# Attention with a shared score tile for the last queries of two heads, and a new order of all engines

## The reference, cut to what matters

```python
batch, n_heads, seq, head_dim = (4, 8, 576, 64)          # float32
scores = scale * np.matmul(q, k.transpose(0, 1, 3, 2))
cum = np.cumsum(np.maximum(s, 0.0), axis=-1)
bias = -(cum[:, :, :, None] - cum[:, :, None, :])
scores = np.where(causal, -1000000000.0, scores + np.minimum(bias, 0.0))
attn = np.exp(scores - np.max(scores, axis=-1, keepdims=True))
attn = attn / (np.sum(attn, axis=-1, keepdims=True) + 1e-09)
return np.matmul(attn, v).astype(np.float32)
```

## Time and profile before

| | us |
|---|---|
| median of 3 runs (lowest, highest) | 879.79 (879.1, 881.36) |
| the profiled execution | 881.97 |
| its span, first to last instruction | 880.2 |
| TensorE busy | 775.4 |
| VectorE busy | 486.0 |
| ScalarE busy | 378.7 |
| GpSimd busy | 163.6 |

### The profile page before, as it was taken

The page is one execution under the profiler, slowest core; times in us unless marked ns, Lnnn a source line. Parts: engine busy times, 40 slices in busy tenths (PEclk is TensorE's granted clock), DMA queues, the critical chain, the costliest instruction groups (busy, mean ns, idle before and its releaser), DMA issues.

```text
span 880.2 us, 15547 instructions
## 1 busy us (share of the span) xinstructions
PE 775.4 (88%) x4885; PEld 649.7 (74%) x4886; DVE 486.0 (55%) x947; ACT 378.7 (43%) x846; POOL 163.6 (19%) x341
## 2 busy tenths in 40 slices
PE   2778888788888999999999997579999999999993
PEld 2566667566676899989899895458888888887772
DVE  8577777877775363453462353854644663726221
ACT  2576676766765340431431512334442551533110
POOL 4134454532222100000000000021122122221121
PEclk9999999999999999999999998579999999999997
DMA  6622232222210000010010012961543561611110
GB/s 156 192 57 57 58 71 54 54 64 57 64 26 23 3 1 1 1 54 0 0 54 0 0 55 71 365 239 38 222 164 119 206 235 49 225 32 34 41 42 16
DMA packets 81405, 70.41 MB, mean 80 GB/s; under 512 B 61960, under 2 KB 61960, under 8 KB 81322
## 3 DMA queue, kind: packets, MB, share of 16 engines
q1 hardware_dynamic: 77354, 58.49, 21.6%
q0 software_dynamic: 4000, 11.28, 3.9%
HBM read 59.72 MB, written 11.86 MB: 81 GB/s over the span
## 4 chain that ended last, share of the span: by engine, by line
PE 82%; DVE 10%; ACT 3%; issue 2%; DMA 1%; SPq 0%; POOL 0%; POOLq 0%; ACTq 0%; DVEq 0%
PE sbank L1091 25%; PE sbank L1684 10%; PE sbank L1686 9%; PE sbank L1685 9%; PE obank L837 5%; PE tbank L806 5%; PE sbank L786 4%; DVE nmax L661 3%; PE sbank L788 3%; PE obank L1139 2%; ACT probs L551 1%; DVE q L653 1%; PE tbank L1669 1%; PE tbank L1709 1%; PE sbank L793 1%
## 5 line engine op out<-in xcount | busy, mean ns | idle before, releaser
L551 ACT ACTIVATE probs<-sbank,nmax 128x128 f32<-128x128 f32 (+4 forms) x160 | 90.6, 568 | 62.3 <-DVE nmax L661 60.8
L806 PE MATMUL tbank<-ident,probs 128*128 128x128 f32 x480 | 75.7, 279 | 20.5 <-ACT pT L558 20.1
L786 PE MATMUL sbank<-k,q 128*128 128x256 f32 (+2 forms) x192 | 74.4, 393 | 16.3 <-ACT probs L551 14.7
L661 DVE TENSOR_REDUCE nmax<-sbank 128x1 f32<-128x128 f32 (+4 forms) x160 | 80.1, 532 | 7.5 <-PE sbank L793 5.9
L1684 PE MATMUL sbank<-w_high,xsT_h 128*128 x184 | 75.0, 407 | 1.9 <-DVE xsT_l L1609 1.7
L1193 DVE TENSOR_TENSOR w_low<-w_low,w_high (+1 forms) x64 | 74.0, 1218 | 0.7 <-ACT w_high L1549 0.3
L1686 PE MATMUL sbank<-w_low,xsT_h 128*128 x184 | 72.7, 395 | 0.0
L1685 PE MATMUL sbank<-w_high,xsT_l 128*128 x184 | 72.5, 394 | 0.0
L1684 PE MATMUL sbank<-w_high,hidT_h 128*128 x176 | 71.0, 403 | 0.1
L806 PEld LDWEIGHTS tbank<-ident,probs 128*128 128x128 f32 x480 | 51.1, 141 | 25.7 <-ACT pT L558 23.9
L1549 ACT CAST w_high<-w_low (+1 forms) x64 | 62.3, 1053 | 17.5 <-SPq L1438 17.5
(11 more groups left out here) (246 smaller groups left out, 1939.7 us busy)
## 6 DMA issues: line engine op xcount, KB each, us to landing
w_low<-in_moe_w_dram SPq DMA_DIRECT2D x16, 2048.0 KB, 14.1
k_raw<-in_k_dram SPq DMA_DIRECT2D x32, 128.0 KB, 2.3
q_raw<-in_q_dram SPq DMA_DIRECT2D x32, 128.0 KB, 2.4
v_raw<-in_v_dram SPq DMA_DIRECT2D x32, 128.0 KB, 2.3
x_dram<-x SPq DMA_DIRECT2D x4, 1024.0 KB, 4.4
win_raw<-in_moe_w_in_dram SPq DMA_DIRECT2D x1, 2048.0 KB, 7.9
wsg_raw<-in_moe_w_sg_dram SPq DMA_DIRECT2D x1, 1152.0 KB, 5.8
wout_raw<-in_moe_w_out_dram SPq DMA_DIRECT2D x1, 1024.0 KB, 10.8
```

Source lines behind the costliest of these rows:

```text
L551: nc.scalar.activation(probs_view(u, i, r), score_view(i, r), ACT.Exp, bias=nmax[u][0:r, i:i + 1], accum_out=sums[(t // 2) % 2][0:r, u, i: ...
L661: nc.vector.tensor_reduce(nmax[u][0:r, i:i + 1], score_view(i, r), ax, ALU.max, negate=True).then_inc(maxed, 1)
L786: nc.tensor.matmul(dst, q1[c][:, q_cols], k1[c][:, cols], start=True, stop=False)
L806: mm = nc.tensor.transpose(tbank[:, n % 2, at:at + P], probs[h % 2][:, OFF_P[i] + P * j:OFF_P[i] + P * (j + 1)], ident[:, :])
```

## The change

- Tiles of 64 queries: the last 64 queries of both heads share one tile of 128 rows, the first head's in rows 0 to 63, the second's below. It is made of eight products of 288 columns: `q1` and `q2` hold zeros in the other head's half, so the heads' products add up. One row maximum, one exponential and five transposes serve both. `probs4`, `pT4` and `mask_last` belong to it; its reciprocals are put on a diagonal (`recip_last`) and turned by a product with `fold`.
- `turn_probs` has three groups a head. `attend(m, 1)` becomes 8 products of 128 columns and 10 of 64.
- ScalarE writes the rounded k of both heads in one instruction on 128 partitions, and the rounded q of both into `q_both`; VectorE writes the remainder of k in one. GpSimd copies to all places that need a copy (`copy_q`, `copy_k`): eight copies of 64x576 for a pair. `load_aug_k` loads four rows of k2 after GpSimd's copy of k2.
- The tails of k and q are loaded into one tile and turned together (`turn_tails`). VectorE and no longer ScalarE copies the main reciprocals (`recips_out`).
- Loops run over `g`, one step for each pair, with pairs g, g-1, g-2 and g-3 in flight. There are semaphores for each tile. The w_sg transposes stand at the end of step 0, and so do memsets of the sets of pair 1 on VectorE. GpSimd splits two shares in each of steps 3 to 10.

```diff
+            def load_aug(m):
+                c, b = sets(m), m % 2
+                sp.dma_start(k2[c + 1][AUG_ROWS[1], :].bitcast(F32), aug_k_dram[2 * m + 1, :, :]).then_inc(aug_in[b], 16)
+                for u in range(2):
+                    sp.dma_start(q2[c + u][AUG_ROWS[u], Q_ALL[u]].bitcast(F32),
+                                 aug_q_dram[2 * m + u, :, BOTH_ALL[u]]).then_inc(aug_in[b], 16)
+            def load_aug_k(m):
+                sp.dma_start(k2[sets(m)][AUG_ROWS[0], :].bitcast(F32),
+                             aug_k_dram[2 * m, :, :]).then_inc(aug_k_in[m % 2], 16)
...
+            sp.wait_ge(k2_copied, 1)
+            load_aug_k(0)
+            sp.wait_ge(late_sets, 4)
+            load_v(0)
             sp.dma_start(win_raw[:, :, :], w_in.rearrange("(k p) n -> p k n", p=P)).then_inc(w_in_landed, 16)
             sp.dma_start(wout_raw[:, :, :], w_out.rearrange("(k p) n -> p k n", p=P)).then_inc(w_out_landed, 16)
...
+            sp.wait_ge(consts, 3)
+            for m in range(1, PAIRS):
+                if m >= 2:
+                    sp.wait_ge(scored[1][3], m - 1)
+                load_aug(m)
+                if m + 1 < PAIRS and m >= 1:
+                    sp.wait_ge(k_turned, m)
                     load_kq(m + 1)
-                if t % 2 == 0 and m >= 2:
-                    sp.wait_ge(av_done[1], m - 1)
-                    load_v(m)
+                sp.wait_ge(k2_copied, m + 1)
+                load_aug_k(m)
+                if m >= 2:
+                    sp.wait_ge(av_done[0], m - 1)
+                load_v(m)
...
+            def copy_q(m, n):
+                c, u = sets(m), n // 2
+                dst = (q1, q2)[n % 2][c + u]
+                return nc.gpsimd.tensor_copy(dst[OWN[u], Q_ALL[u]], q_flat[OWN[u], BOTH_ALL[u]].bitcast(F32))
+            def copy_k(dst, rows, src, src_rows):
+                return nc.gpsimd.tensor_copy(dst[rows, :], src[src_rows, :].bitcast(F32))
...
+                c = sets(m)
+                if alive(m):
+                    if m == 1:
+                        pool.wait_ge(consts, 3)
+                    pool.wait_ge(tails_high, m + 1)
+                    copy_q(m, 1).then_inc(q_copied, 1)
+                    copy_q(m, 2).then_inc(q_copied, 1)
+                    copy_q(m, 3).then_inc(q_copied, 1)
+                if alive(g - 2):
...
+                        pool.wait_ge(widened, 3 * (g - 2))
+                    widen(g - 2)
+                if alive(m):
+                    pool.wait_ge(k_low, m + 1)
+                    copy_k(k2[c + 1], BOTTOM, k2[c], BOTTOM).then_inc(k2_copied, 1)
+                    copy_k(k1[c + 1], TOP, k1[c], BOTTOM).then_inc(k1_copied, 1)
+                    copy_q(m, 0).then_inc(q_copied, 1)
+                    copy_k(k1[c + 1], BOTTOM, k1[c], BOTTOM).then_inc(k1_copied, 1)
+                    pool.wait_ge(k1_copied, 3 * m + 2)
+                    copy_k(k1[c], BOTTOM, k1[c], TOP).then_inc(k1_copied, 1)
...
+            def split_q(m):
+                act.wait_ge(q_turned, m + 1)
+                if m:
+                    act.wait_ge(q_copied, 4 * m)
+                nc.scalar.mul(q_flat[:, BOTH_MAIN], obank[:, 1, :], SCALE).then_inc(q_high, 1)
+            def split_tails(m):
+                act.wait_ge(tails_turned, m + 1)
+                nc.scalar.copy(k1[sets(m)][:, TAIL], obank[:, 1, 0:LAST])
+                nc.scalar.mul(q_both[:, 0:2 * ST:2 * ST - 1, :],
+                              obank[:, 1, LAST:2 * LAST].unsqueeze(1).to_broadcast([P, 2, D]),
+                              SCALE).then_inc(tails_high, 1)
+            def split_k(m):
+                act.wait_ge(k_turned, m + 1)
+                nc.scalar.copy(k1[sets(m)][:, MAIN], obank[:, 0, :]).then_inc(k_high, 1)
...
+            for g in range(PAIRS + 2):
+                if alive(g):
+                    split_q(g)
+                if alive(g - 2):
+                    last_exps(g - 2)
+                    exps(1, 3, g - 2)
+                    probs_out(0, 2, g - 2)
+                    probs_out(1, 1, g - 2)
+                if alive(g):
+                    split_tails(g)
+                if alive(g - 1):
+                    exps(0, 0, g - 1)
+                    exps(0, 1, g - 1)
+                if alive(g - 2):
+                    last_probs_out(g - 2)
+                if alive(g):
+                    split_k(g)
+                if alive(g - 1):
+                    exps(0, 2, g - 1)
+                    if g >= 2:
+                        act.wait_ge(turned[1][0], g - 1)
+                    exps(1, 0, g - 1)
+                if alive(g - 2):
+                    probs_out(1, 0, g - 2)
+                if alive(g - 1):
+                    exps(1, 1, g - 1)
+                    exps(0, 3, g - 1)
+                    exps(1, 2, g - 1)
+                    probs_out(0, 1, g - 1)
...
+                nc.vector.memset(q2[u][:, :].bitcast(F32), 0.0)
+                nc.vector.memset(q1[u][:, Q_ZERO[u]].bitcast(F32), 0.0).then_inc(consts, 1)
+            nc.vector.memset(k2[1][TOP, :].bitcast(F32), 0.0)
...
+            for g in range(PAIRS + 3):
+                if alive(g - 2):
+                    last_row_max(g - 2)
+                    row_max(1, 3, g - 2)
+                if alive(g):
+                    low_q(g, 0)
+                    low_q(g, 1)
+                if alive(g - 3):
+                    output(g - 3, 0)
+                if alive(g - 2):
+                    invert(g - 2)
+                if alive(g - 1):
+                    row_max(0, 0, g - 1)
+                    row_max(0, 1, g - 1)
+                if alive(g - 2):
+                    probs_out(1, 2, g - 2)
+                if alive(g):
+                    low_tails(g)
+                if alive(g - 1):
+                    row_max(0, 2, g - 1)
+                    row_max(1, 0, g - 1)
+                    row_max(0, 3, g - 1)
+                    row_max(1, 1, g - 1)
+                if alive(g):
+                    low_k(g)
+                if alive(g - 2):
+                    recip_tail_out(g - 2)
+                if alive(g - 1):
+                    row_max(1, 2, g - 1)
+                if alive(g - 2):
+                    recips_out(g - 2)
+                    output(g - 2, 1)
+                if alive(g - 1):
+                    probs_out(0, 0, g - 1)
...
+                    for u in range(2):
+                        nc.vector.memset(q2[2 + u][:, :].bitcast(F32), 0.0)
+                        nc.vector.memset(q1[2 + u][:, Q_ZERO[u]].bitcast(F32), 0.0)
+                    nc.vector.memset(k2[3][TOP, :].bitcast(F32), 0.0).then_inc(consts, 1)
...
+            def score(dst, c, q_cols, k_cols, first, last):
+                nc.tensor.matmul(dst, q1[c][:, q_cols], k1[c][:, k_cols], start=first, stop=False)
+                return nc.tensor.matmul(dst, q2[c][:, q_cols], k2[c][:, k_cols], start=False, stop=last)
+            def scores(u, i, m):
+                c = sets(m) + u
+                at = Q_MAIN[u].start + P * i
+                w = max(W_P[i], 2 * P)
+                score(sbank[:, i, 0:w], c, slice(at, at + P), slice(0, w), True, False)
+                nc.tensor.matmul(sbank[:, i, P * i:P * (i + 1)], ident_bf[:, :], mask_bf[:, :], start=False,
+                                 stop=True).then_inc(scored[u][i], 1)
+            def last_scores(m):
+                for a in range(2):
+                    for u in range(2):
+                        score(sbank[:, a, 0:HALF], sets(m) + u, Q_LAST[u], slice(a * HALF, (a + 1) * HALF),
+                              u == 0, u == 1 and a == 0)
+                nc.tensor.matmul(sbank[:, 1, HALF - LAST:HALF], ident_bf[:, :], mask_last[:, :], start=False,
+                                 stop=True).then_inc(last_scored, 1)
+            def turn_probs(u, n, m):
+                for at, (j, i) in enumerate(GROUPS_OF[n]):
+                    mm = turn(tbank[:, n % 2, P * at:P * (at + 1)],
+                              probs[u][:, OFF_P[i] + P * j:OFF_P[i] + P * (j + 1)])
+                if (u, n) == (1, 1):
+                    mm = turn(tbank[:, 1, 3 * P:4 * P], probs4[:, FULL * P:SP])
+                mm.then_inc(turned[u][n], 1)
...
+            def turn_recip_tail(m):
+                nc.tensor.matmul(tbank[:, 1, 0:LAST], recip_last[:, :], fold[:, :], start=True,
+                                 stop=True).then_inc(recip_tail_turned, 1)
+            def attend(m, c):
+                v = v_raw[m % 2]
+                pt = [pT[(2 * m + u) % 3] for u in range(2)]
+                if c == 0:
+                    for j, at in enumerate([GROUP_AT[0], GROUP_AT[1], GROUP_AT[1] + 2 * P]):
+                        for u in range(2):
+                            mm = nc.tensor.matmul(obank[OWN[u], 0, P * j:3 * P], v[:, j, u, :],
+                                                  pt[u][:, at:at + (3 - j) * P], start=(j == 0), stop=(j == 2))
...
+                    for j in range(FULL):
```

(86 more changed lines are left out.)

655 lines of the change are left out of this document (225 added, 430 removed).

## The result

The changed kernel takes 825.35 us (median, 824.19 to 827.3), the kernel before, beside it on the same chip, 880.58 us (879.1 to 881.59): a ratio of 0.9376, with an interval of 0.9352 to 0.94. The profiled execution of the changed kernel took 827.3 us (span 825.5), 54.67 us less than that of the kernel before. The forecast was 837.0, a gain of 45.0, with a range of 829 to 859. The direction was right; the size was 9.7 us short, and the median lies 3.65 us under the low end of the range.

A forecast was written before the change was run, and what follows sets the result against it. TensorE was taken to bound the kernel, with 13.31 us of work and 2.59 of idling a pair. Steps of 13.0 would end attention at 238.9 instead of 283.9 us, 45.0 less: 881.97 to 837.0, range 829 to 859.

The forecast's parts named there:

- the walk: One loop step followed through TensorE's order: everything it waits for is ready 0.7 us or more before it is wanted.
- 12.93: TensorE's own work for one pair in the new loop, in us, with ends 12.6 and 13.4.
- The start, 13.31: TensorE's work for a pair in the old loop, 15.90 x 25.11/30 us, leaving 2.59 us of idling.
- The edits: TensorE's changes per pair: seven transposes fewer -0.77, one mask product fewer -0.03, fold +0.22, short attend products +0.20 us.
- The hand-offs, 0.07: Passing work between engines in the loop, which took a step from 12.93 to 13.0 us.
- rival 1: Short products of attend(m, 1) bound by weight loads: 1.04 a pair instead of 0.20, total 850 us; chance 0.12.
- Prologue and fill: Before full steps: first row maximum near 27.3 us, step 1 6.3, step 2 12.0, plus 1 us for slow TensorE.
- SyncE's ring: Loop loads of augmented k rows: 6.7 us available against 128 KB loads that land in 2.3.
- Rival 3: TensorE stays at its slow rate through step 2: 7 us more, total 844; chance 0.09 together with the GpSimd case.
- Rival 4: Augmented-row loads exceed their 6.7 us and lengthen 15 steps: 894 us at 10.5 us of landing; chance 0.03.
- drain 10.8 for 10.3: End of attention: step 17 takes 8.2 us to the reciprocals, then attend(15, 0) and its output 2.1.
- the low case of 829.8: Low end of the range: 12.7 us a step by the lower bounds and 3 us off the fill.

The follow-up runs named there:

- e1: Changed kernel with the four transposes of the reciprocals issued twice for each pair: 833.03 us, ratio to the kernel before 0.9453.
- e7: Changed kernel with four extra 64x576 copies on GpSimd for each pair, ahead of its copy of k2: 837.52 us, ratio to the kernel before 0.95.
- e4: Changed kernel with the five memsets of the second pair's sets moved from VectorE to GpSimd: 824.73 us.
- f2: Changed kernel, second execution with memsets on GpSimd and pair 2's q and k and pair 1's augmented rows loaded ahead of the MLP weights: 825.31 us, ratio 0.9361.
- f1: Changed kernel once more, with no edit, beside the next run on the same chip: 824.88 us, ratio to the kernel before 0.9365.
- e5: Changed kernel with pair 2's k and q loads issued ahead of the 3 MB of MLP weights: 823.66 us, ratio to the kernel before 0.9349.
- e6: Changed kernel, first execution with memsets on GpSimd and pair 2's q and k and pair 1's augmented rows loaded ahead of the MLP weights: 824.12 us, ratio 0.9359.

## Why the prediction was right in sign and short in size

**What bounds the loop: right.** The two waits of the earlier trace rows are gone, none took their place, and TensorE is the bound (e1). No margin of the walk was used up, the smallest of 0.7 to 1.0 us included: no wait shows in the loop.

**TensorE's work of a pair: 12.19 and not 12.93.** This is the step of the prediction that failed, a term of the sum that was mis-sized, in two ways.
- The start, 13.31 = 15.90 x 25.11/30, was 0.26 too high. The busy share holds the drains ahead of the two waits, 0.24 and 0.16, which go with the waits. From start to start the work was 13.05 in the kernel before. (That makes 0.40, of which 0.14 is taken back: each stretch of 30 us holds both waits twice but only 1.89 periods, so its share puts idle time at 2.59 a pair where the waits are 2.45.) The prediction took all that is not idle for work.
- The edits give -0.86 and not -0.38. Start to start over whole steps of both traces: transposes of probabilities 3.31 to 2.57, of k, q and tails 1.01 to 0.87, reciprocals with `fold` 0.60 to 0.69, scores and masks 5.13 to 5.02, attend 3.01 to 3.05. Take the fold's 0.25 out, and the seven transposes that go give 1.04 where 0.77 was forecast: 0.15 each, not the 0.11 of a row of four. Part of the rest is in the changes from one group of transposes straight to another. Before, five probabilities ahead of the tails take 0.60, four ahead of k 0.49, four ahead of the reciprocals 0.47, and one reciprocal ahead of the other four 0.16: 0.18 in all over 0.11 each. After, the two such changes cost 0.02. That leaves 0.11 of the 1.04 without a place, and the reading is argued from the spacings and not tried; e1, which put four transposes behind four others in one group, paid 0.11 each. Scores gained 0.11 for 0.03.
- The hand-offs, 0.07, are not there: nothing in the step waits.

**The short products: rival 1 is out.** The second half of attend, TensorE's timeline of after:

```profile
103.99 1.09 PE L853 MATMUL obank<-pT,v_raw 128*64 128x128 f32 x16
104.91 0.75 PE L858 MATMUL obank<-pT,v_raw 128*64 128x64 f32 x20
105.59 0.43 PE L838 MATMUL tbank<-fold,recip_last 128*128 128x64 f32 x2
105.83 0.42 PE L800 MATMUL sbank<-k,q 128*128 128x384 f32 x1
```

From 104.91 to 105.59 are ten record pairs, 0.068 us each, between the 0.055 of width alone and the 0.137 of the rival. The half is 105.59 - 103.99 = 1.60 against the 1.56 of the earlier trace rows, so +0.04 where I took 0.20. By the rule of the Trainium skill ("TensorE: Matmul & The Clock Gate", LDWEIGHTS) the two heads' loads in turn would need 107 ns a pair; the trace has 68, so here they overlap. The fold takes 0.25, for 0.22.

**The other engines: right enough.** VectorE is busy 24.97/30 x 12.19 = 10.1 us a step (10.4 forecast), ScalarE 9.0 (8.7), GpSimd 6.0 and 9.7 with weights (6.5 and 10.3). GpSimd's copies, by line in after:

```profile
L496 POOL CAST q<-q_both 64x576 fp32r<-64x576 f32 x64 | 41.7, 665 | 59.0 <-ACT q_both L568 57.1
```

At 0.665 us for 576 columns they go at the loop's rate of before (0.69 forecast by width), not at the 0.85 for 512 of the earlier trace rows. Those two copies did not run beside memsets, as the prediction read it. VectorE's timeline of before, and then the same instruction in after, where GpSimd is idle from 3.9 to 12.93:

```profile
10.87 1.10 DVE L627 TENSOR_TENSOR aug<-cum,aug 32x576 f32<-32x576 f32 x1
```

```profile
8.88 0.75 DVE L652 TENSOR_TENSOR aug<-cum,aug 32x576 f32<-32x576 f32 x1
```

VectorE was on an instruction with two SBUF inputs, and on two more of the running sum. Both engines were slower there: the copies took 0.85 for 0.61, VectorE 1.10 for 0.75 and then 0.86 and 0.85 for 0.44 and 0.44. The rule of the Trainium skill ("GPSIMD Engine Reference", Specifications) names two SBUF inputs of VectorE as one case of contention; the trace of before agrees, and so does the loop of after, where the copies kept their rate. What I missed there is the time between GpSimd's instructions: e7 puts its need at 10.8 a step, 1.1 over its busy time. With the shorter step, 12.19 for 13.0, its room is 1.4 us and not the 2.6 that I gave it.

**Prologue and fill: right by chance.** TensorE's timeline of after has the transposes of w_sg at 12.99 (14.5 forecast), and VectorE's the first row maximum at 25.12 (27.3 forecast). The running sum takes 3.8 us where the prediction kept the 4.9 of before, because GpSimd's copies no longer run beside it:

```profile
12.99 2.69 PE L942 MATMUL sbank<-ident,wsg_raw 128*128 128x128 f32 x10
...
25.12 0.62 DVE L683 TENSOR_REDUCE nmax<-sbank 128x1 f32<-128x128 f32 x2
```

The 2.2 us gained there went again. Step 2 starts at 36.07, 1.78 of it a wait for pair 2's loads, which SyncE issues behind 3 MB of weights; the rest of step 1 took 36.07 - 1.78 - 25.12 = 9.2 us where I put 6.3. Some 1.8 of these 2.9 us go with TensorE's rate. Here are the products of 384 columns in step 1, in after and then in e4 (the memsets alone):

```profile
30.26 0.69 PE L800 MATMUL sbank<-k,q 128*128 128x384 f32 x1 [0.69 <-ACT probs L579]
```

```profile
29.78 0.44 PE L800 MATMUL sbank<-k,q 128*128 128x384 f32 x1 [0.94 <-ACT probs L583]
```

In after the rate is the slow one until about 33.4 us; in e4 and f2 it is the full one by 30 us. The same stretch of step 1 takes 7.4 us in these two, and 9.1 to 9.4 in after, f1, e5 and e6, where it is slow. The prediction put 1 us for the slow rate, and put it into step 2. Step 2 then took 47.56 - 36.07 = 11.5 where I put 13.0 with TensorE's lower rate. So -2.2 + 2.9 + 1.8 - 1.5 = +1.0, four misses that nearly cancel. I weighed SyncE's ring only for the loop, and had no wait for these loads. Rival 3 is out: four transposes take 0.63 us at 47.56 as in the loop, and step 2 is no longer than its work. Rival 4 is out: no load makes the loop wait.

**The sum, redone.** A pair gives 15.90 - 12.19 = 3.71 us: 2.45 of idle time, 0.40 of drains and 0.86 of TensorE's work. The prediction had 2.9 of it. Thirteen steps of 12.19 and one of 11.30 are 169.8 where 182 stood. Of the 12.2 us, 0.81 x 14 = 11.3 is the size of a step; 0.9 is step 16, which I counted as a full one, though its nine transposes of k and q are missing. Fill +1.0, drain 10.8 for 10.3: 12.2 - 1.0 - 0.5 = 10.7 early, and 1.0 more after attention leaves 9.7. That 1.0 lies within what one execution differs from the next: the same later stages take 597.3 us in the second execution of the changed kernel (824.49 - 226.6 - 0.56) and 596.4 to 598.6 in its edits of the fill.

**The range.** Its low end took 12.7 a step, by the lower bounds of the edits on top of 13.31. No bound was put on the 13.31 itself, which was the largest term. With 13.05 there and all else as it was, the low case of 829.8 would have been 829.8 - 14 x 0.26 = 826.2, under the 827.3 of the profiled execution and within a microsecond of the median.

## What to carry to other kernels

Take TensorE's work from the distance between starts in a stretch without waits, not from its busy share: each of the two waits here had a drain ahead of it, 0.24 and 0.16 us, that was counted as busy and went when the wait went. Where an engine has two waits in a period, moving one step in the queue that feeds it may give little (0.13 of 15.9 us here): a new wait and longer spacings took back the rest of the 0.8; ask for the period that all queues allow. And before an engine is given more, test its room with dummy work: 2.86 us of copies showed that GpSimd's spare time was 1.4 us a step, where its busy share promised 12.19 - 9.7 = 2.5.

## What was unexpected of the hardware

- The two waits on TensorE have 0.16 and 0.24 us in front of them that the profile counts as busy and that an unwaited product doesn't need.
- Ten products of 64 columns in a row, each with a weight load of its own that is recorded at 0.138 us, follow each other in 0.068 us a record pair. Transposes in f32 are 0.11 us apart with loads of 0.141.
- The clock column can miss a slow stretch. In after each product of 256 columns at 22 to 29 us starts 0.36 us ahead of the next, as in e6, and 0.20 at 38.55. In e6 the granted clock of that stretch is 0.50 (1.2 GHz); in after the column reads 1.00.
- Four of SyncE's six load issues behind the 3 MB of weights took 1.77 to 2.31 us, and in the next step five of six 0.40 to 0.61. SyncE's timeline of after, with the same load behind 3 MB of weights and then without:

```profile
26.93 2.31 SPq L405 DMA_DIRECT2D k_raw<-in_k_dram  x1
...
38.27 0.40 SPq L405 DMA_DIRECT2D k_raw<-in_k_dram  x1
```

- In the fill the same edit gave a last output at 225.1 us in one execution and 226.9 in another, and the changed kernel 227.6 and 226.6. In the one with 226.9 the granted clock fell to half behind a wait of 1.49 us that followed others of 0.69 and 0.44; in e6 it stayed up behind one of 1.07. The one with 225.1 had also begun the transposes of pair 1's q 1.05 us earlier, at 20.55. A gain of 2 us in a stretch that varies like this may not last.
